# One batch's attention moved into the token mix and output projection of the batch before it

## The chip, the cores and the metric

The kernel runs on one core of a Trainium2 chip. The metric is device time in microseconds (us), median of three runs. The core's engines are TensorE (PE, matrix products), VectorE (DVE), ScalarE (ACT), GpSimd (POOL) and SyncE (SP, which here only issues DMAs). Each engine works through its own list of instructions in order; semaphores tie the lists together.

## The reference

Three stages over 4 batches of 576 tokens, all in fp32:

```
x = softmax(q k^T / 8 + mask) v          # 8 heads of 64; heads 0-3: the last 32 keys,
                                         # heads 4-7: keys of the same class mod 32, causal
h = gelu(x @ w_in); u, v = halves(h)     # 512 -> 512 + 512
v = layernorm(v) * g
x = x + (u * (w_sg @ v + b_sg)) @ w_out  # w_sg mixes the 576 tokens
x = x + relu(layernorm(x) * g2 @ w1) @ w2   # 512 -> 2048 -> 512
```

## The kernel before

Phase A loops over the batches; phase B (the last line above) then runs over six tiles of 384 tokens, for all batches together, and isn't changed. A product is done as three in fp32r (`split_product`, L839 to L841): high by high, high by low, low by high, so that each operand exists as a rounded part (`..._hi`, made by a copy) and a remainder (`..._lo`, made by a subtraction, mostly on POOL).

Phase A for one batch, as PE's list has it:

- Attention, in 22 blocks: a local block has 96 queries and 128 keys, a strided one up to 7 residue classes (126 queries, 126 keys; the last of each pair 72). A block holds the two heads of a pair. `scores` (L857, L858) first adds the mask into PSUM by a bf16 product with the identity, then multiplies the queries, with all 128 rows (two heads of 64), by keys stored twice with zeros in the other head's rows, 256 columns in fp32. `maxima` (DVE, L653) takes both row maxima, `exps` (ACT, L474) the exponentials with row sums, `normalise` (DVE, L660, L664) divides, `transposes` (PE, L869) turns both heads, `copy_pT` (ACT, L485) brings them to SBUF, `values` (PE, L883) multiplies by all 128 columns of v and `copy_low`, `copy_high` (L670, L491) keep the half of each head that is wanted. Queries are scaled by ACT beforehand (L466). Scores run three blocks ahead, and values two blocks behind.
- `v_part`: the v half of w_in, 5 groups of 12 products of 512 columns; then 8 `u` groups, 8 `mix` groups (14 products of 288 columns) and 8 `out` groups (12 of 288). ACT and DVE empty them (`gelu_v`, `gelu_u`, `gate`, `add_out`); DVE and POOL normalise v in between.
- The eight PSUM banks are shared in time: four for scores, two for transposes, two for values; then all eight for the groups.

PE's list for a batch is: attention (the first v products between its last blocks), v, u, mix, out, with the first three score blocks of the next batch between the last out groups. In the last batch, the mean of tile 0 of phase B (`mean_product`, L947) follows the u groups. POOL has summed the four chunks for it by then: it does so (`sum_x`, L368, L372) as soon as the last values product is done, ahead of the v normalisation. SP loads the next batch's q, k and v when a batch's last values product is done.

Of the kernel before, what the change touches and what calls it, by code (L numbers as in the profile page):

```python
# [16 lines left out]
F32 = mybir.dt.float32  # L17
# [6 lines left out]
P = 128  # L24
B, H, S, D = 4, 8, 576, 64
DM = H * D
# [16 lines left out]
CLASSES = P // CLASS  # L43
SB = CLASSES * CLASS
# [8 lines left out]
for _pair in range(PAIRS // 2, PAIRS):  # L53
    for _r in range(0, STRIDE, CLASSES):
        _n = min(CLASSES, STRIDE - _r) * CLASS
        BLOCKS.append((_pair, _n, _n, _r * CLASS, STRIDE + _r * CLASS, 2))
NT = len(BLOCKS)


# [10 lines left out]
GROUP_BANK = [(NT - 4 + i) % 4 for i in range(4)] + [4] + 3 * list(range(8))  # L70
NGELU = NS + 2 * GC
NMIX = 2 * GC
W_PARTS = (slice(0, KC * P), slice(KC * P, KC * P + DM))
NOUT = 2 * KC
WIN_SPLIT = (9, 11, 13, 15)
EARLY = 3
DVE_W2 = (0, 1, 2, 8, 9)


def sequence_block_kernel(nc, qT, kT, vW, w_in, g1, w_sgT, b_sg, w_out, g2, w_ff, masks, eye, out):  # L80
    with ExitStack() as ctx:
# [15 lines left out]
        k_sb = sb("k_sb", [P, PAIRS, 2, KPAD], F32, phase_a)  # L97
        v_sb = sb("v_sb", [P, NT, P], F32, phase_a)
        win_hi = sb("win_hi", [P, KC, 2 * GATE], F32R, phase_a)
        win_lo = sb("win_lo", [P, KC, 2 * GATE], F32R, phase_a)  # L100
        eye_b = sb("eye_b", [P, P], BF16, phase_a)
        mask_b = sb("mask_b", [P, 3, 2 * P], BF16, phase_a)
# [5 lines left out]
        op_hi = sb("op_hi", [P, KC, S], F32R, phase_a)  # L108
        op_lo = sb("op_lo", [P, KC, S], F32R, phase_a)
        stat = sb("stat", [P, 3, 2 * NT], F32, phase_a)  # L110
        neg_max, row_sum, row_inv = (stat[:, i, :].rearrange("p (t h) -> p t h", h=2) for i in range(3))
# [6 lines left out]
        with ExitStack() as raw:  # L118
            win_raw = sb("win_raw", [P, KC, 2 * GATE], F32, raw)

        res_by_chunk = res[:].rearrange("p (c t) -> p c t", c=KC)
        wout_raw = res_by_chunk[:, :, S:S + DM]
        wsg_raw = res_by_chunk[:, :, 2 * S:3 * S]
        wsg_raw_last = res[:, 3 * S:4 * S]
        mask_raw = res[:, BS + 3 * S:BS + 3 * S + 3 * P]
        u_sb = sb("u_sb", [P, GC, S], F32, phase_a)
        vn_hi = sb("vn_hi", [P, NS, GATE], F32R, phase_a)
        vn_lo = sb("vn_lo", [P, NS, GATE], F32R, phase_a)
        gt = sb("gt", [P, 3, HALF], F32, phase_a)

        with ExitStack() as attention:
            probs = sb("probs", [P, 4, 2 * P], F32, attention)
            probsT = sb("probsT", [P, 2, 2 * P], F32, attention)
        gv = sb("gv", [P, 3, GATE], F32, phase_a)
        phase_a.close()

# [31 lines left out]
        s_bank, t_bank, o_bank = bank[0:4], bank[4:6], bank[6:8]  # L168
# [5 lines left out]
        q_scaled = sem("q_scaled")  # L174
        k_zero = sem("k_zero")
# [13 lines left out]
        x_low, x_high = sem("x_low"), sem("x_high")  # L189
        x_hi, x_lo = sem("x_hi"), sem("x_lo")  # L190
        xe_lo = sem("xe_lo")
# [32 lines left out]
        def res_at(b, chunk, first, n, p0=0, p1=P):  # L224

            return res[p0:p1, bass.ds(b * S + (chunk * BS + first), n)]
# [9 lines left out]
        def head_out(b, t, low):  # L236

            pair, nq, _, q0, _, m = BLOCKS[t]
            p0, p1 = (0, D) if low else (D, P)
            src = o_bank[t % 2][p0:p1, 0:nq] if low else o_bank[t % 2][p0:p1, nq:2 * nq]  # L240
            if m != 2:
                return res_at(b, pair, q0, nq, p0, p1), src

            r0, nr = q0 // CLASS, nq // CLASS
            dst = res_at(b, pair, 0, S, p0, p1).rearrange("p (a r) -> p r a", r=STRIDE)[:, r0:r0 + nr, :]
            return dst, src.rearrange("p (r a) -> p r a", a=CLASS)

# [8 lines left out]
        def res_count(b, i):  # L258

            return b * NOUT + (NOUT + 2 + i)  # L260

        def blocks_upto(pair):
            return sum(1 for blk in BLOCKS if blk[0] <= pair)

        @block.sync
        def _(sp):
            def load_qkv(b, first=False):
                for pair in range(PAIRS):
                    sp.dma_start(q_sb[:, pair, :], qT[b, :, pair, :]).then_inc(q_in[pair], 16)
                    if first and pair == 0:  # L270
                        sp.dma_start(mask_raw, masks).then_inc(mask_in, 16)
                        sp.dma_start(eye_f[:], eye).then_inc(mask_in, 16)
                    for h in range(2):
                        rows = slice(D * h, D * h + D)
                        sp.dma_start(k_sb[rows, pair, h, :], kT[b, rows, pair, :]).then_inc(k_in[pair], 16)  # L275
                    blocks = slice(blocks_upto(pair - 1), blocks_upto(pair))
                    sp.dma_start(v_sb[:, blocks, :], vW[b, :, blocks, :]).then_inc(v_in[pair], 16)
# [10 lines left out]
            with sp.Fori(1, B) as b:  # L288
                sp.wait_ge(pv_ready, b * NT)
                load_qkv(b)  # L290


            sp.wait_ge(pv_ready, B * NT)
# [15 lines left out]
        def _(pool):  # L309
# [3 lines left out]
            pool.wait_ge(k_zero, 2)  # L313
            pool.memset(k_sb[0:D, 1:, 1, :], 0.0).then_inc(k_zero, 1)
            pool.wait_ge(k_zero, 3)
            pool.memset(k_sb[D:P, 1:, 0, :], 0.0).then_inc(k_zero, 1)

            def split_weights(part):

                if part < KC:  # L320
                    pool.wait_ge(win_hi_ready, part + 1)
                    lo, raw_, hi = win_lo[:, part, :], win_raw[:, part, :], win_hi[:, part, :]
                else:
                    i = part - KC
                    if i < NS - 2:
                        pool.wait_ge(wrest_hi_ready, i + 1)
                        lo, raw_, hi = wsg_lo[:, i, :], wsg_raw[:, i, :], wsg_hi[:, i, :]
                    else:
                        i -= NS - 2
                        pool.wait_ge(wrest_hi_ready, NS + i + 1)  # L330
                        lo, raw_, hi = wout_lo[:, i, :], wout_raw[:, i, :], wout_hi[:, i, :]
                pool.tensor_tensor(lo, raw_, hi.bitcast(F32), ALU.subtract).then_inc(wa_lo, 1)

            def split_x(b, pair):
                pool.wait_ge(x_hi, b * PAIRS + (pair + 1))
                settle(pool)
                pool.tensor_tensor(op_lo[:, pair, :], res_at(b, pair, 0, S), op_hi[:, pair, :].bitcast(F32),  # L337
# [12 lines left out]
            def split_v(b, s):  # L350
                pool.wait_ge(vnh_ready, b * NS + (s + 1))
                pool.tensor_tensor(vn_lo[:, s, :], gv[:, s % 3, :], vn_hi[:, s, :].bitcast(F32),
                                   ALU.subtract).then_inc(vnl_ready, 1)

            def split_gated(b, i):
                _, c, h = GROUPS[NGELU + i]
                pool.wait_ge(gh_ready, b * NMIX + (i + 1))
                pool.tensor_tensor(op_lo[:, c, h * HALF:(h + 1) * HALF], gt[:, i % 3, :],
                                   op_hi[:, c, h * HALF:(h + 1) * HALF].bitcast(F32),
# [35 lines left out]
            def batch(b, first=False, last=False):  # L395
                if first:
                    for part in range(KC):
                        split_weights(part)
                for pair in range(PAIRS - 1):
                    split_x(b, pair)  # L400
                if last:
                    pool.wait_ge(pv_ready, B * NT)
                    pool.memset(xc[:, 0:P], 1.0 / DM).then_inc(b_const, 1)
# [712 lines left out]
```

## Time and profile before

| | us |
|---|---|
| three runs | 764.59, 765.59, 766.84 (median 765.59) |
| the profiled execution | 764.36 |
| its span, first to last instruction | 761.8 |
| PE busy in the span | 739.5 (97%), mean granted clock 0.996 |
| DVE, ACT, POOL busy | 337.4, 275.0, 198.0 |
| first attention product | 6.56 |
| u products of batch 0 start | 59.3 |
| phase B starts | 352.2 |

Busy time of PE counts the pipelined length of each product, so neighbours overlap: what a product costs is the distance between two starts. The stages can be told by the tiles that a product reads: `k_sb`, `probs`, `probsT` are attention, `win` with 512 columns v, with 288 columns u, `wsg` mix, `wout` out. A half-speed stretch shows in PEclk, and in durations.

### The profile page before, as it was taken

The page shows a single profiled execution, that of the slowest core. Times are in us where ns is not written, and L with a number is a line of the kernel's source. Part 1 is how long each engine was busy: PE and PEld are TensorE (multiplying, and loading weights), DVE is VectorE, ACT ScalarE, POOL GpSimd, SP SyncE. Part 2 cuts the span into 40 slices and gives each one's busy share as a digit, 9 for nine tenths or more (in the row PEclk, how much of TensorE's full clock was granted, in tenths as well). Part 3 has the DMA queues.
Part 4 walks back from the last instruction along what each step waited for, and adds up shares of the span by engine and source line. Part 5 has one row for each costly group of instructions (what it writes and reads, how often), then busy time and mean ns, then how long its engine had stood idle before and what let it go on. Part 6 is the DMA issues. An engine that isn't in the chain of part 4 may idle for free.

```text
span 761.8 us, 12255 instructions
## 1 busy us (share of the span) xinstructions
PE 739.5 (97%) x4400; PEld 693.0 (91%) x4400; DVE 337.4 (44%) x736; ACT 275.0 (36%) x826; POOL 198.0 (26%) x190
## 2 busy tenths in 40 slices
PE   6798999999999999999999999999999999999998
PEld 4578986899679977999999999999999999999998
DVE  5955667635854486675453223223122322222112
ACT  6663458425952386352442122121112211211110
POOL 1518602530124203655434021111302031110000
PEclk9899999999999999999999999999999999999999
DMA  8525000600042001011330100100010010001001
GB/s 254 223 65 141 1 0 1 203 0 0 0 134 69 0 1 51 7 64 68 119 122 18 42 1 1 41 1 1 1 42 1 1 43 1 0 1 42 1 1 41
DMA packets 15227, 34.34 MB, mean 45 GB/s; under 512 B 1872, under 2 KB 5200, under 8 KB 15184
## 3 DMA queue, kind: packets, MB, share of 16 engines
q1 hardware_dynamic: 15184, 33.76, 14.0%
q8 instruction: 27, 0.44, 0.2%
q14 instruction: 16, 0.13, 0.1%
HBM read 29.04 MB, written 4.72 MB: 44 GB/s over the span
## 4 chain that ended last, share of the span: by engine, by line
PE 88%; DVE 3%; issue 3%; ACT 2%; DMA 2%; SPq 1%; POOL 0%; DVEq 0%; ACTq 0%
PE bank L839 26%; PE bank L841 26%; PE bank L840 26%; PE bank L883 3%; PE bank L858 2%; PE bank L869 2%; DMA win_raw<-w_in_dram 1%; ACT probs L474 1%; DVE probs L664 1%; DVE stat L653 1%; PE bank L857 1%; SPq L275 1%; PE bank L942 1%; PE bank L941 1%; DMA w_raw<-w_ff_dram 0%
## 5 line engine op out<-in xcount | busy, mean ns | idle before, releaser
L802 DVE SCALAR_TENSOR_TENSOR hid_lo<-bank,hid_hi 128x384 fp32r<-128x384 f32 x96 | 53.5, 557 | 282.8 <-ACT hid_hi L604 282.8
L604 ACT ACTIVATE hid_hi<-bank 128x384 fp32r<-128x384 f32 x96 | 47.1, 491 | 298.1 <-PE bank L841 298.1
L839 PE MATMUL bank<-xn_hi,w_hi 128*128 128x384 f32 x384 | 129.1, 336 | 1.2 <-DVE res L711 1.2
L840 PE MATMUL bank<-xn_lo,w_hi 128*128 128x384 f32 x384 | 129.5, 337 | 0.0
L841 PE MATMUL bank<-hid_hi,w_lo 128*128 128x384 f32 x384 | 129.5, 337 | 0.0
L839 PE MATMUL bank<-hid_hi,w_hi 128*128 128x384 f32 x384 | 129.4, 337 | 0.0
L841 PE MATMUL bank<-xn_hi,w_lo 128*128 128x384 f32 x384 | 129.2, 336 | 0.0
L840 PE MATMUL bank<-hid_lo,w_hi 128*128 128x384 f32 x384 | 128.9, 336 | 0.0
L474 ACT ACTIVATE probs<-bank,stat 96x128 f32<-96x128 f32 (+2 forms) x176 | 61.7, 355 | 38.3 <-DVE stat L653 36.9
L839 PEld LDWEIGHTS bank<-xn_hi,w_hi 128*128 128x128 f32 x384 | 72.1, 188 | 1.4 <-DVE res L711 1.4
L839 PEld LDWEIGHTS bank<-hid_hi,w_hi 128*128 128x128 f32 x384 | 72.2, 188 | 0.0
L841 PEld LDWEIGHTS bank<-xn_hi,w_lo 128*128 128x128 f32 x384 | 72.1, 188 | 0.0
L840 PEld LDWEIGHTS bank<-hid_lo,w_hi 128*128 128x128 f32 x384 | 72.1, 188 | 0.0
L840 PEld LDWEIGHTS bank<-xn_lo,w_hi 128*128 128x128 f32 x384 | 72.1, 188 | 0.0
L841 PEld LDWEIGHTS bank<-hid_hi,w_lo 128*128 128x128 f32 x384 | 72.0, 188 | 0.0
L858 PE MATMUL bank<-k_sb,q_sb 128*96 128x256 f32 (+2 forms) x176 | 54.2, 391 | 0.0
L664 DVE TENSOR_TENSOR probs<-probs,stat 96x256 f32<-96x256 f32 (+2 forms) x88 | 49.8, 566 | 3.0
L883 PE MATMUL bank<-probsT,v_sb 128*128 128x192 f32 (+2 forms) x176 | 50.2, 371 | 0.6 <-DVE res L670 0.2
L869 PEld LDWEIGHTS bank<-eye_f,probs 96*128 96x128 f32 (+2 forms) x176 | 20.5, 142 | 32.4 <-DVE probs L664 14.4
L392 POOL TENSOR_TENSOR xn_lo<-xc,xn_hi 128x1536 fp32r<-128x1536 f32 x6 | 21.0, 3506 | 103.4 <-ACT xn_hi L544 103.4
L337 POOL TENSOR_TENSOR op_lo<-res,op_hi 128x576 fp32r<-128x576 f32 x12 | 17.1, 1424 | 115.1 <-DVE op_hi L677 115.1
L869 PE MATMUL bank<-eye_f,probs 96*128 96x96 f32 (+2 forms) x176 | 33.6, 273 | 8.4 <-DVE probs L664 4.1
(101 smaller groups left out, 1454.1 us busy)
## 6 DMA issues: line engine op xcount, KB each, us to landing
w_raw<-w_ff_dram SPq DMA_DIRECT2D x16, 512.0 KB, 3.5
k_sb<-kT_dram SPq DMA_DIRECT2D x32, 152.0 KB, 5.0
q_sb<-qT_dram SPq DMA_DIRECT2D x16, 288.0 KB, 5.6
out_dram<-res SPq DMA_DIRECT2D x5, 768.0 KB, 3.9
v_sb<-vW_dram SPq DMA_DIRECT2D x8, 384.0 KB, 4.6
v_sb<-vW_dram SPq DMA_DIRECT2D x8, 320.0 KB, 6.6
win_raw<-w_in_dram SPq DMA_DIRECT2D x4, 512.0 KB, 10.2
res<-w_sgT_dram SPq DMA_DIRECT2D x1, 1152.0 KB, 13.3
```

The source lines that it names most:

```text
L337: pool.tensor_tensor(op_lo[:, pair, :], res_at(b, pair, 0, S), op_hi[:, pair, :].bitcast(F32), ALU.subtract).then_inc(x_lo, 1)
L392: pool.tensor_tensor(xn_lo[h][:], xc[:], xn_hi[h][:].bitcast(F32), ALU.subtract).then_inc(xnl_ready, 1)
L474: last = act.activation(probs[0:nq, t % 4, h * nk:(h + 1) * nk], s_bank[t % 4][0:nq, h * nk:(h + 1) * nk], ACT.Exp, bias=neg_max[0:nq, t, ...
L604: act.activation(hid_hi[:, f % 2, :], h_bank[f % 2][:, 0:TILE], ACT.Relu).then_inc(hh_ready, 1)
L664: dve.tensor_tensor(e, e, inv, ALU.mult).then_inc(probs_ready, 1)
L802: dve.scalar_tensor_tensor(out=hid_lo[:, f % 2, :], in0=h_bank[f % 2][:, 0:TILE], scalar=0.0, in1=hid_hi[:, f % 2, :].bitcast(F32), op0=AL ...
L839: pe.matmul(dst, wh, xh, start=(start and i == 0), stop=False)
L840: pe.matmul(dst, wh, xl, start=False, stop=False)
L841: last = pe.matmul(dst, wl, xh, start=False, stop=(stop and i == n - 1))
L858: pe.matmul(dst, q_sb[:, pair, q0:q0 + nq], k_sb[:, pair, :, k0:k0 + nk], start=False, stop=True).then_inc(scores_ready, 1)
L869: last = pe.transpose(t_bank[t % 2][0:nk, h * nq:(h + 1) * nq], probs[0:nq, t % 4, h * nk:(h + 1) * nk], eye_f[0:nq, 0:nq])
L883: pe.matmul(o_bank[t % 2][:, 0:2 * nq], v_sb[0:nk, t, :], probsT[0:nk, t % 2, 0:2 * nq], start=True, stop=True).then_inc(pv_ready, 1)
```

## The change

Blocks come in twins: 24 blocks (strided ones now hold 6 or 5 classes, 108 or 90 queries), 12 twins of two blocks, three twins to each pair. The attention of batch 0 runs alone ("solo"). The attention of batch b+1 runs within the mix and out groups of batch b, in 14 steps: a step has the scores of twin s, the transposes of twin s-2, a mix or out group, the values of twin s-2, and in two steps a second group. The last batch has its products alone.

Scores are now one product per head and block, with 64 of the array's rows (rows 0 to 63 for one head, 64 to 127 for the other) and 128, 108 or 90 key columns. Values are one product per head and block, with 64 of the array's columns, so each head's result lands in its own half of the partitions. The mask product, the doubled keys, their zeroing, and the scaling of the queries go. Instead DVE does, per head and block, one `tensor_tensor_reduce` from PSUM that adds the mask, scales, writes to SBUF and takes the maximum; and ACT's exponentials read SBUF. The normalisation is four `tensor_scalar` per twin. In the interleaved steps, attention uses banks 0 to 3 (one set) and the groups banks 4 to 7; solo has two sets.

```diff
-            def scores(b, t):
...
-                pe.matmul(dst, eye_b[0:nq, 0:nq], mask, start=True, stop=False)
-                pe.matmul(dst, q_sb[:, pair, q0:q0 + nq], k_sb[:, pair, :, k0:k0 + nk],
-                          start=False, stop=True).then_inc(scores_ready, 1)
+            def scores(b, s, solo=False):
+                if solo and s >= 2:
+                    pe.wait_ge(max_ready, b * NT + 2 * (s - 1))
+                if not solo and s >= 1:
+                    pe.wait_ge(max_ready, b * NT + 2 * s)
...
+                for j in range(2):
+                    pair, nq, nk, q0, k0, _ = BLOCKS[2 * s + j]
+                    for h in range(2):
+                        rows = slice(h * D, (h + 1) * D)
+                        last = pe.matmul(scores_at(s, j, h, solo), q_sb[rows, pair, q0:q0 + nq],
+                                         k_sb[rows, pair, k0:k0 + nk], start=True, stop=True)
+                last.then_inc(scores_ready, 1)
...
+            def values(b, s, solo=False):
...
+                for j in range(2):
+                    for h in range(2):
+                        rows = slice(h * D, (h + 1) * D)
+                        last = pe.matmul(values_at(s, solo)[rows, j * nq:(j + 1) * nq], v_sb[0:nk, 2 * s + j, rows],
+                                         probsT[0:nk, (2 * j + h) * nq:(2 * j + h + 1) * nq], start=True, stop=True)
+                last.then_inc(pv_ready, 1)
```

DVE:

```diff
+            def maxima(b, s, solo=False):
...
+                for j in range(2):
+                    mask = mask_b[0:nq, BLOCKS[2 * s + j][5], 0:nk]
+                    for h in range(2):
+                        last = dve.tensor_tensor_reduce(out=probs_at(s, j, h), in0=scores_at(s, j, h, solo),
+                                                        in1=mask, scale=-SCALE, scalar=3.0e38, op0=ALU.add,
+                                                        op1=ALU.min, accum_out=stat_at(neg_max, s, j, h))
...
+            def normalise(b, s):
...
+                for j in range(2):
+                    for h in range(2):
+                        e = probs_at(s, j, h)
+                        last = dve.tensor_scalar(e, e, stat_at(row_inv, s, j, h), None, ALU.mult)
+                last.then_inc(probs_ready, 1)
```

PE while the next batch's attention is interleaved:

```diff
+            def period(b, first=False):
+                projections(b, first)
+                for s in range(STEPS):
+                    if s < TWINS:
+                        scores(b + 1, s)
+                    if s >= LAG:
+                        transposes(b + 1, s - LAG)
+                    for i in AFTER_T[s]:
+                        group(b, NGELU + i, first)
+                    if s >= LAG:
+                        values(b + 1, s - LAG)
+                    for i in AFTER_P[s]:
+                        group(b, NGELU + i, first)
```

PE in solo, then DVE in solo:

```diff
+            for s in range(STEPS):
+                if LAG <= s:
+                    transposes(0, s - LAG, solo=True)
+                if s < TWINS:
+                    scores(0, s, solo=True)
+                if LAG <= s:
+                    values(0, s - LAG, solo=True)
...
+            for s in range(STEPS):
+                if s < TWINS:
+                    maxima(0, s, solo=True)
+                if 1 <= s <= TWINS:
+                    normalise(0, s - 1)
```

POOL in the last batch:

```diff
+            def last_period(b):
+                split_all_v(b)
+                pool.wait_ge(group_ready, b * len(GROUPS) + NGELU)
+                pool.memset(xc[:, 0:P], 1.0 / DM).then_inc(b_const, 1)
+                pool.memset(eps_c[:], EPS).then_inc(b_const, 1)
+                pool.wait_ge(b_const, 2)
+                pool.tensor_copy(mean_w[:], xc[:, 0:P]).then_inc(b_const, 1)
+                sum_x(0)
+                split_sum(0, False)
```

The v products run batch by batch in one piece, over the four chunks of their input; `gv` and `gt` get a buffer for every group instead of three.

## Rows read from the trace of the kernel before

**Rows 1.** The page's busy time, share of the span and instructions, by engine.

```profile
PE 739.5 (97%) x4400; PEld 693.0 (91%) x4400; DVE 337.4 (44%) x736; ACT 275.0 (36%) x826; POOL 198.0 (26%) x190
```

**Rows 2.** Windows: length, then busy us (instructions) by engine, granted clock, DMA.

```profile
6.56:12.20 5.64, 5.64 (x17) 3.88 (x18) 3.16 (x10) 3.34 (x16) 0.00 (x0) 1.00 1.00 275
...
21.50:25.70 4.20, 2.32 (x13) 1.31 (x11) 4.17 (x9) 2.92 (x13) 1.84 (x2) 1.00 1.04 405
25.70:31.70 6.00, 5.24 (x18) 3.94 (x19) 5.90 (x12) 3.81 (x18) 4.02 (x2) 0.53 0.71 249
...
34.00:42.90 8.90, 6.32 (x34) 4.00 (x33) 8.73 (x24) 6.25 (x28) 5.32 (x3) 1.00 0.00 0
42.90:59.30 16.40, 16.40 (x78) 12.94 (x78) 7.99 (x23) 8.31 (x24) 3.84 (x6) 1.00 0.39 110
59.30:71.90 12.60, 12.60 (x96) 12.58 (x95) 9.62 (x15) 7.18 (x15) 11.26 (x13) 1.00 0.66 168
71.90:74.60 2.70, 0.29 (x3) 0.06 (x1) 0.00 (x0) 0.41 (x1) 2.52 (x2) 1.00 0.00 0
...
186.40:210.50 24.10, 22.94 (x131) 16.05 (x129) 21.57 (x74) 21.61 (x102) 2.80 (x2) 1.00 0.00 0
...
226.90:309.40 82.50, 81.75 (x520) 70.61 (x519) 50.43 (x139) 44.39 (x160) 26.00 (x33) 1.00 0.12 36
```

**Rows 3.** Timeline of PE, batch 1: one local block; columns start us, us, engine, line.

```profile
108.10 0.27 PE L857 MATMUL bank<-mask_b,eye_b 96*96 96x256 bf16 x1
108.21 0.59 PE L858 MATMUL bank<-k_sb,q_sb 128*96 128x256 f32 x2
108.65 0.33 PE L869 MATMUL bank<-eye_f,probs 96*128 96x96 f32 x2
108.81 0.52 PE L883 MATMUL bank<-probsT,v_sb 128*128 128x192 f32 x2
```

**Rows 4.** Timeline of PE, batch 3: the first products of two mix groups.

```profile
322.42 0.29 PE L839 MATMUL bank<-wsg_hi,vn_hi 128*128 128x288 f32 x1
...
324.29 0.29 PE L839 MATMUL bank<-wsg_hi,vn_hi 128*128 128x288 f32 x1
```

**Rows 5.** Timeline of PE, batch 0: from 128 to 64 weight columns in v.

```profile
56.33 0.39 PE L841 MATMUL bank<-win_hi,op_lo 128*128 128x512 f32 x1
56.56 0.40 PE L839 MATMUL bank<-win_hi,op_hi 128*64 128x512 f32 x1
```

**Rows 6.** Timeline of DVE: normalising a block, a scaling, six out groups added.

```profile
105.02 0.15 DVE L660 RECIPROCAL stat<-stat 96x2 f32<-96x2 f32 x1
105.21 0.42 DVE L664 TENSOR_TENSOR probs<-probs,stat 96x256 f32<-96x256 f32 x1
105.55 0.41 DVE L653 TENSOR_REDUCE stat<-bank 96x2 f32<-96x256 f32 x1
...
142.56 0.55 DVE L688 TENSOR_SCALAR gv<-gv,mean_var,rstd_v 128x512 f32<-128x512 f32 x1 [0.16 <-POOL rstd_v L347]
...
346.98 2.27 DVE L711 TENSOR_TENSOR res<-bank,res 128x288 f32<-128x288 f32 x6
```

**Rows 7.** Timeline of ACT: an accumulator read and the operation after it.

```profile
105.40 0.19 ACT L474 ACTIVATION_READ_ACCUMULATOR probs<-bank,stat 96x1 f32 x1
105.49 0.35 ACT L474 ACTIVATE probs<-bank,stat 96x128 f32<-96x128 f32 x1
```

**Rows 8.** Timeline of PE and DVE at the start.

```profile
5.22 1.01 DVE L641 CAST mask_b<-res 128x384 bf16<-128x384 f32 x2 [2.89 <-DMA eye_f<-eye_dram]
6.77 1.06 PE L858 MATMUL bank<-k_sb,q_sb 128*96 128x256 f32 x2
```

**Rows 9.** Timeline of POOL, batch 3: preparing the mean of tile 0.

```profile
301.12 0.20 POOL L403 MEMSET xc<- 128x128 f32 x1 [3.73 <-PE bank L883]
...
304.65 1.01 POOL L372 TENSOR_TENSOR acc<-acc,res 128x384 f32<-128x384 f32 x1 [0.18 <-POOL acc L372]
...
319.28 1.01 POOL L387 TENSOR_TENSOR acc_lo<-acc,acc_hi 128x384 fp32r<-128x384 f32 x1
```

More of the change, by code:

```diff
@@ L272, in load_qkv @@
                         sp.dma_start(eye_f[:], eye).then_inc(mask_in, 16)
[L273 to L276, printed above, removed]
+                    blocks = slice(2 * PER_PAIR * pair, 2 * PER_PAIR * (pair + 1))
                     sp.dma_start(v_sb[:, blocks, :], vW[b, :, blocks, :]).then_inc(v_in[pair], 16)
@@ L393, in split_xn, with split_all_v @@
                                    ALU.subtract).then_inc(xnl_ready, 1)
[L395 to L403, printed above, removed]
-                    pool.memset(eps_c[:], EPS).then_inc(b_const, 1)
-                    pool.wait_ge(b_const, 2)
-                    pool.tensor_copy(mean_w[:], xc[:, 0:P]).then_inc(b_const, 1)
-                    sum_x(0)
+            def split_all_v(b):
                 root_v(b, 0)
@@ L549, in weights_hi, with gelus @@
                     act.activation(w_hi[f][:, part], w_raw[:, f % 2, part], ACT.Copy).then_inc(wff_hi, 1)
[L551 to L561 removed]
+            def gelus(b, first=False, last=False):
                 for s in range(NS):
@@ L598, in _ @@
+            period(0, first=True)
             with act.Fori(1, B - 1) as b:
-                batch(b)
-            batch(B - 1, last=True)
+                period(b)
+            last_period(B - 1)
             def hidden_hi(n, f):
@@ L796, in _ @@
+            round_x(0, PAIRS - 1)
+            period(0, first=True)
             with dve.Fori(1, B - 1) as b:
-                batch(b)
-            batch(B - 1, last=True)
+                period(b)
+            last_period(B - 1)
             def hidden_lo(n, f):
@@ new lines, in transposes @@
+            def transposes(b, s, solo=False):
+                _, nq, nk, _, _, _ = BLOCKS[2 * s]
+                if solo and s >= 2:
+                    pe.wait_ge(pT_copied, b * TWINS + (s - 1))
+                if not solo and s >= 1:
+                    pe.wait_ge(pT_copied, b * TWINS + s)
+                pe.wait_ge(probs_ready, b * TWINS + (s + 1))
+                settle(pe)
+                for j in range(2):
+                    for h in range(2):
+                        cols = slice((2 * j + h) * nq, (2 * j + h + 1) * nq)
+                        last = pe.transpose(transposed_at(s, solo)[0:nk, cols], probs_at(s, j, h), eye_f[0:nq, 0:nq])
+                last.then_inc(pT_ready, 1)
```

600 lines of the change are left out of this document (294 added, 306 removed).

## The prediction

> **What bounds the kernel now.** I read the page's busy line first: PE 97%, DVE 44% [rows 1]. The other engines could be slower without harm as long as PE has work, so the question is what PE does and where it stands still. Windows by stage answer it [rows 2]: a batch in the middle, from u products to u products (226.9 to 309.4), takes 82.5 us, 81.75 of them busy. Its attention stretch (186.4 to 210.5, 24.1 us) is also busy, with ACT and DVE at 21.6 us beside it. So little idle time is there to be filled: of the 82.5 us under 1.5. What the change can save is PE's own work in attention.
>
> That work is what is left when the dense products are taken off. v: 60 products at 0.23 [rows 5] = 13.8; u: 12.6 for its 96 [rows 2]; mix: 8 groups at 1.87 [rows 4] = 15.0; out: 96 like u = 12.6. Together 54.0, so attention costs 82.5 - 54.0 = 28.5 us a batch, stalls included.
>
> **Attention inside a period (three times).** From starts in one block [rows 3]: the mask product 0.11; 256 fp32 columns 0.44, which is 1.7 ns a column; two transposes 0.16. The mask products go. A local twin (two blocks) has 4 score products of 128 columns, 4 x 128 x 1.7 ns = 0.87; 4 value products of 96, 0.65; 4 transposes, 0.32: in all 1.84. A strided twin has 96 columns in the mean: 0.65 + 0.65 + 0.32 = 1.62. Six of each: 20.8 us if the halves of the array take turns. Columns set a product's time, not rows, and there are as many as before; so halving the rows pays only if two halves work at once. If they always do, scores and values halve: 6 x 1.08 + 6 x 0.97 = 12.3 us. No row shows two products at once. I take the middle, 16.5, because a head's products come in its own order (each fp32 product is two instructions), so that only neighbours of different heads can meet.
>
> Between shapes of the array (64 rows, full, 64 columns, and back) there are 4 changes a step, 48 a period. The nearest row has none: going from 128 to 64 weight columns in v, the next product starts after the usual 0.23 [rows 5]. The other end is that the array empties each time: a product of 288 columns lasts 0.29 and the next group's rhythm is 1.87/14 = 0.13 [rows 4], a tail of 0.16. I take 0.05, nearer to the row: 2.4 us; and 1.6 us for waits that come late. So 20.5 us instead of 28.5: 8.0 less a period, 24.0 in three. Bounds: 12.3 (16 less) to 20.8 + 48 x 0.16 + 1.6 = 30.1 (1.6 more).
>
> The Trainium skill, page "TensorE: Matmul & The Clock Gate", section "Part 3: Packing small matmuls — row/col tiling", says products in different row groups run concurrently, and gives 3.07 times for four row tiles. By that the attention would be near 14 us; the trace of before can't show it.
>
> Does PE get its inputs? The steps hold 27.6 us of mix and out, so 27.6 + 20.5 = 48 us of PE in 14 steps, some 3.5 each. DVE in them: the new mask-and-maximum operation, 48 times. Not in the trace; an addition from PSUM of 288 columns takes 2.27/6 = 0.38 [rows 6], so 128 columns about 0.20, plus an accumulator read, for which ACT's is 0.09 from start to start [rows 7]: 0.29, strided 0.26, in all 13.2. Bounds 0.15 (no separate read, two columns at once) and 0.6 (two passes). Normalising: reciprocal 0.19 to the next start, and four scalings; one of 512 columns lasts 0.55 [rows 6], so 128 columns 0.17 to 0.36; I take 0.23 from start to start: 1.1 a twin, 13.2. Copies of results 1.8, rounding 1.7, gates 8 x 0.9 (two operations of 288 columns) = 7.2, out additions 8 x 0.4 = 3.2. Sum 40.3, under 48. ACT has less: per twin four exponentials at 0.35 [rows 7], two copies, near 2. Each wait in a step (transposes for last step's normalising, values for this step's copy behind a group, scores for last step's maxima) is answered a product group earlier. So PE sets the pace here, and DVE could lag a little without harm. v and u in four banks instead of eight lose nothing: ACT is busy 7.2 of the 12.6 us in which the u groups run [rows 2].
>
> **Solo attention (batch 0).** Before, it and v end at 59.3 [rows 2]. In the new order PE issues the transposes of twin s-2 ahead of the scores of twin s, the transposes wait for the normalising that DVE does last in step s-1, and DVE's next maxima wait for those scores. So nothing overlaps in the ring DVE to PE to DVE: maxima 1.1 + normalising 1.1 + PE's 0.32 transposes, 0.65 scores, 0.16 tail, 0.2 for changes and signals = 3.55 us a step. Before, two of the 22 blocks took (42.9 - 6.6)/11 = 3.3 in the mean [rows 2], with scores three blocks ahead. At half clock PE's part doubles by 1.07: 4.6. PE's real share would be (0.32 + 0.65 + 0.5)/3.55 = 41%. The window 21.5 to 25.7, with busy 2.32 of 4.2, was followed by a granted clock of 0.53; one with 6.32 of 8.9 kept 1.00 [rows 2]. So the clock should be low for part of it. Its first products run slow anyway: 1.06 for a pair that later lasts 0.59 [rows 3, 8]. I take 4.1, ten rings = 41.
>
> Start 5.4 (the identity lands at 5.2 [rows 8]; the zeroing and the query scaling that went took no path time but about 1 us), first scores, maxima, exponentials and normalising to 10.5, + 41 = 51.5, + 5.0 for the last two twins' transposes, copies and values, none of which v products fill any more = 56.5, + v 13.8 + 1.5 at half clock = 71.8. Against 59.3: 12.5 more. Bounds: rings of 3.2 (3.5 more) and of 4.9 (21 more). POOL's four remainders of w_in no longer hit DVE's path: they run while DVE waits for PE.
>
> **First mix of batch 0.** PE stands 2.4 of 2.7 us now [rows 2], for POOL's remainders of v and w_sg. With five v buffers the gelus don't wait and the scores come in between: 1.5 less. Bounds 0 to 2.4.
>
> **Last batch.** POOL's sum for tile 0 now waits for all u groups. From memset to sum it was 301.12 to 305.66 [rows 9] = 4.5; ACT's rounding 0.5, signals 0.2, remainder 1.0 [rows 9] = 6.2. PE has `mean_product` next in its list, so everything behind it, mix and out, waits: 6 us that weren't there. After such a stop the clock should be low for a while; the start lost 5.64/2 = 2.8 that way [rows 2]. I take 8.5 in all; bounds 4 and 10. The next stop, var_product before mix 6, has its input after some 10 us, as late as PE gets there.
>
> **Sum.** -24.0 + 12.5 - 1.5 + 8.5 = -4.5 on the profiled execution's 764.4: 759.9. The median of the runs is 1.2 above it: 761. Phase B isn't touched, and its weights land earlier.
>
> **Rivals.**
> 1. Halves overlap fully: attention 12.3 + 2 = 14.3 us, 14 less a period, and rings of 3.2: -42.6 + 3.5 - 1.5 + 8.5 = -32: 733. For it: the two heads' operands share no rows or banks. Against: the order within a head.
> 2. Slower: solo's ring. It stays at half clock with rings of 4.9 and ends 21 later, and periods save 7.0 each: -21 + 21 - 1.5 + 9 = +7.5: 773. For it: the half clock of 25.7 to 31.7, after 55% busy [rows 2]. Against: at half clock PE is at 60% and may rise. It decides once ten rings and the end cost more than the periods save less 7, that is from rings of 4.6 on with 8 a period.
> 3. The halves take turns and each change empties the array (0.16): periods lose 1.6 each, solo another 3: +4.8 + 15.5 - 1.5 + 8.5 = +27: 793. Against it: no loss in [rows 5], though that row may not be such a change. The Trainium skill, page "TensorEngine Tiling (Array Packing)", section "Key Properties", says that changing the tiling mode drains TensorE; that speaks against this change, and no row here shows its price.
> 4. DVE becomes the bound. At 0.6 a mask-and-maximum costs 28.8 a period, DVE's sum 56 against 48: 8 x 3 - 24 = 0 there, solo another 12.5: 25 - 1.5 + 8.5 = +32: 798. It decides from (48 - 27.1)/48 = 0.44 on. Against: the sum above.
>
> **Chances.** Forecast 0.38 (its own range 751 to 770); rival 1 0.19; rival 2 0.20; rival 3 0.12; rival 4 0.11. About 0.3% (2.3 us) is what can be told from no change. Faster: most of the first (0.28), rival 1, a little of rival 2: 0.49. Same: 0.10. Slower: 0.41. The range leaves out the far ends of rivals 1, 3 and 4: 739 to 787.
>
> **What would show it.** Start of u in batch 0 near 72, with PE idle in every solo step waiting for DVE's scaling, and PEclk below 10 there. From u to u in the middle near 74.5 us. Starts of a twin's eight score instructions: 0.87 (turns) or 0.43 (both) in all, and a longer gap at the changes if the array empties. PE standing 6 us ahead of L947's successor in the last batch. Wrong: PE waiting for DVE's maxima inside the periods, a solo under 45 us, or a period above 80.

## The result, and the profile after

The changed kernel takes 767.05 us (median of 20 runs, 765.28 to 769.75), the kernel before 765.62 in the same rounds (20 runs, 764.27 to 766.84): ratio 1.0023, 95% interval 1.0013 to 1.0032. It is slower by 0.1 to 0.3%; the forecast was 761, faster. The profiled executions took 767.55 and 764.36, with spans of 765.8 and 761.8. The table goes by them. They are 3.2 us apart, the medians 1.4; the rest is the scatter of single executions.

| stretch, us | before | after | difference | predicted |
|---|---|---|---|---|
| start to u of batch 0 | 59.3 | 79.5 | +20.2 | +12.5 |
| u of batch 0 to u of batch 3 | 250.1 | 223.8 | -26.3 | -25.5 |
| u of batch 3 to phase B | 42.8 | 52.8 | +10.0 | +8.5 |
| phase B | 409.6 | 409.7 | +0.1 | 0 |
| span | 761.8 | 765.8 | +4.0 | -4.5 |

The busy line of the page after, which answers [rows 1]:

```profile
PE 720.7 (94%) x4744; PEld 681.1 (89%) x4744; DVE 328.5 (43%) x1024; ACT 253.0 (33%) x738; POOL 198.0 (26%) x192
```

PE is busy 19 us less in a span that is 4 longer: it stands still more. Windows of the changed kernel, in the columns of [rows 2], say where:

```profile
11.38:54.50 43.12, 28.82 (x212) 20.97 (x212) 24.67 (x144) 22.97 (x98) 8.05 (x4) 1.00 0.36 137
54.50:60.04 5.54, 0.00 (x1) 0.03 (x1) 5.44 (x4) 0.48 (x1) 5.38 (x4) 1.00 0.00 0
...
155.70:229.60 73.90, 73.72 (x607) 64.95 (x606) 49.40 (x212) 38.33 (x138) 23.33 (x28) 1.00 0.16 56
...
316.00:322.00 6.00, 0.21 (x3) 0.05 (x1) 0.00 (x0) 0.93 (x2) 4.46 (x7) 0.93 0.00 0
322.00:326.00 4.00, 4.00 (x16) 4.00 (x17) 1.75 (x1) 0.94 (x2) 0.14 (x1) 0.50 0.00 0
```

In a middle batch PE is busy 73.72 of 73.90 us, as the plan of the change has it. (The 1.00 in the first row doesn't show it, but products last nearly twice as long there: eight score instructions 1.10 us, in a period 0.61.) The cost is in solo attention, where 54.50 to 60.04 has no product at all while DVE and POOL are both busy, and in the last batch (316 to 322).

**The stop at the end of solo.** Timelines of PE, DVE and POOL of the changed kernel there:

```profile
60.04 0.80 PE L924 MATMUL bank<-eye_f,probs 90*90 90x90 f32 x4 [5.54 <-issue]
63.20 0.77 PE L891 MATMUL bank<-win_hi,xop_hi 128*128 128x512 f32 x1 [0.82 <-issue]
```

```profile
51.28 0.79 DVE L701 TENSOR_SCALAR probs<-probs,stat 90x90 f32<-90x90 f32 x4
...
53.51 6.43 DVE L701 TENSOR_SCALAR probs<-probs,stat 90x90 f32<-90x90 f32 x4
```

The same four, one by one, from shorter windows of the same view:

```profile
53.51 2.37 DVE L701 TENSOR_SCALAR probs<-probs,stat 90x90 f32<-90x90 f32 x1
55.80 1.43 DVE L701 TENSOR_SCALAR probs<-probs,stat 90x90 f32<-90x90 f32 x1
57.16 1.43 DVE L701 TENSOR_SCALAR probs<-probs,stat 90x90 f32<-90x90 f32 x1
58.51 1.43 DVE L701 TENSOR_SCALAR probs<-probs,stat 90x90 f32<-90x90 f32 x1
```

```profile
53.48 2.34 POOL L346 TENSOR_TENSOR win_lo<-win_raw,win_hi 128x1024 fp32r<-128x1024 f32 x1 [5.83 <-DVE win_hi L676]
55.77 4.11 POOL L362 TENSOR_TENSOR xop_lo<-res,xop_hi 128x576 fp32r<-128x576 f32 x3
```

The same four scalings take 0.79 us once and 6.43 the next time. The second set began as POOL's last remainder of w_in did and ended at 59.94, when POOL's three remainders of x were done (59.88). One by one, each scaling starts 0.03 us after one of POOL's four operations (53.48, 55.77, 57.13, 58.48) and ends 0.06 after it: each waits for a whole operation of POOL's, and POOL's next one starts just ahead of DVE's next. The transposes wait for the last scaling.

**A step inside a period** (PE; the attention of batch 1 within the mix groups of batch 0: a mix group ends, values, scores, transposes, the next group begins), and DVE's maxima in it:

```profile
112.08 0.29 PE L1006 MATMUL bank<-wsg_hi,vn_hi 128*128 128x288 f32 x1
112.21 0.29 PE L1007 MATMUL bank<-wsg_hi,vn_lo 128*128 128x288 f32 x1
112.43 0.55 PE L940 MATMUL bank<-probsT,v_sb 128*64 128x96 f32 x8
112.91 0.68 PE L909 MATMUL bank<-k_sb,q_sb 64*96 64x128 f32 x8
113.52 0.55 PE L924 MATMUL bank<-eye_f,probs 96*128 96x96 f32 x4
113.86 0.38 PE L891 MATMUL bank<-wsg_hi,vn_hi 128*128 128x288 f32 x1
```

```profile
110.48 0.28 DVE L688 CUSTOM_DVE_ANT_0 probs<-bank,mask_b 96x128 f32<-96x128 f32 x1
110.69 0.08 DVE L688 DVE_READ_ACCUMULATOR2_ANT stat<- 96x1 f32 x1
110.69 0.28 DVE L688 CUSTOM_DVE_ANT_0 probs<-bank,mask_b 96x128 f32<-96x128 f32 x1
```

Read the starts: eight score instructions 0.61 us (112.91 to 113.52), eight value instructions 0.48, four transposes 0.34. In turns they would be 0.87 and 0.65, with full overlap 0.43 and 0.33: they lie between. At the first change of shape, from the mix product of 112.21 to the values, the next start comes after 0.22 instead of the 0.13 that is usual between products of 288 columns: 0.09. In the kernel before, where the array stays whole, this place has the usual 0.13 (97.37 to 97.50, an out product and then a mask product).

Behind the transposes the first mix product also holds up the next one (0.21, 113.86 to 114.07, as in the step before, 110.39 to 110.61). But transposes and mix both use the whole array, and the kernel before has such a delay too, where no shape changes. Its PE behind a score product:

```profile
97.86 0.48 PE L839 MATMUL bank<-op_hi,wout_hi 128*128 128x288 f32 x1
98.18 0.30 PE L840 MATMUL bank<-op_lo,wout_hi 128*128 128x288 f32 x1
```

0.32 instead of 0.13. So this delay isn't a price of the halves; what makes it stays open. The DVE operation goes from start to start in 0.21, its read under the next one.

**The last batch.** PE of the changed kernel; the second row is the first mix product, which lasts 0.44 us where that of [rows 4] lasts 0.29:

```profile
321.98 0.66 PE L1012 MATMUL bank<-acc_hi,mean_w 128*128 128x384 f32 x1 [5.79 <-POOL acc_lo L412]
...
322.75 0.44 PE L891 MATMUL bank<-wsg_hi,vn_hi 128*128 128x288 f32 x1
...
348.91 0.40 PE L891 MATMUL bank<-gated_hi,wout_hi 128*128 128x288 f32 x1 [2.03 <-DVE res L748]
```

and DVE ahead of that second stop:

```profile
343.69 2.55 DVE L766 RECIPROCAL rstd<-rstd 128x384 f32<-128x384 f32 x1 [0.21 <-ACT rstd L566]
346.28 2.21 DVE L772 SCALAR_TENSOR_TENSOR xc<-xc,g2c,rstd 128x384 f32<-128x384 f32 x4
348.40 1.54 DVE L748 TENSOR_TENSOR res<-bank,res 128x288 f32<-128x288 f32 x4
```

The first stop was predicted. The second wasn't: out groups now have four banks, and DVE's additions, which free them, are queued behind the normalising of tile 0.

### The profile page after: what moved, and what is told of

Read it like the earlier page. It is cut to its first block, busy times and chain, and to the rows that moved or that the text cites. A ratio compares the mean times of both kernels' runs of the same rounds, so it can differ in the third digit from the quotient of the medians.

```text
span 765.8 us, 12852 instructions
## 1 busy us (share of the span) xinstructions
PE 720.7 (94%) x4744; PEld 681.1 (89%) x4744; DVE 328.5 (43%) x1024; ACT 253.0 (33%) x738; POOL 198.0 (26%) x192
## 4 chain that ended last, share of the span: by engine, by line
PE 91%; issue 4%; DVE 3%; ACT 1%; POOL 1%; DMA 1%; SPq 0%; DVEq 0%; POOLq 0%; ACTq 0%
PE bank L891 27%; PE bank L892 26%; PE bank L893 26%; PE bank L909 4%; PE bank L924 3%; PE bank L940 3%; DVE probs L701 1%; DVE probs L688 1%; DMA eye_f<-eye_dram 1%; PE bank L1006 0%; PE bank L1007 0%; DVE rstd L766 0%; PE bank L1012 0%; PE bank L1013 0%; DVE xc L772 0%
## 5 line engine op out<-in xcount | busy, mean ns | idle before, releaser
L501 ACT ACTIVATE probs<-probs,stat 96x128 f32<-96x128 f32 (+2 forms) x192 | 71.9, 378 | 17.4 <-DVE stat L688 17.3
L688 DVE CUSTOM_DVE_ANT_0 probs<-bank,mask_b 96x128 f32<-96x128 f32 (+2 forms) x192 | 41.0, 266 | 37.6 <-PE bank L909 34.6
L701 DVE TENSOR_SCALAR probs<-probs,stat 96x128 f32<-96x128 f32 (+2 forms) x192 | 50.9, 324 | 1.8
L924 PE MATMUL bank<-eye_f,probs 96*128 96x96 f32 (+2 forms) x192 | 29.7, 286 | 23.1 <-issue 17.7
L924 PEld LDWEIGHTS bank<-eye_f,probs 96*128 96x128 f32 (+2 forms) x192 | 19.7, 151 | 30.6 <-issue 26.8
L384 POOL TENSOR_TENSOR gated_lo<-u_sb,gated_hi 128x288 fp32r<-128x288 f32 x32 | 27.0, 846 | 61.8 <-ACT gated_hi L547 61.8
L891 PE MATMUL bank<-wsg_hi,vn_hi 128*128 128x288 f32 x128 | 41.0, 320 | 1.7 <-issue 1.7
```

Of the source, the lines that this page charges most:

```text
L384: pool.tensor_tensor(gated_lo[:, c, cols], u_sb[:, c, cols], gated_hi[:, c, cols].bitcast(F32), ALU.subtract).then_inc(gl_ready, 1)
L501: last = act.activation(probs_at(s, j, h), probs_at(s, j, h), ACT.Exp, scale=-1.0, bias=stat_at(neg_max, s, j, h), accum_out=stat_at(row_s ...
L688: last = dve.tensor_tensor_reduce(out=probs_at(s, j, h), in0=scores_at(s, j, h, solo), in1=mask, scale=-SCALE, scalar=3.0e38, op0=ALU.add, ...
L701: last = dve.tensor_scalar(e, e, stat_at(row_inv, s, j, h), None, ALU.mult)
L891: pe.matmul(dst, wh, xh, start=(start and i == 0), stop=False)
L924: last = pe.transpose(transposed_at(s, solo)[0:nk, cols], probs_at(s, j, h), eye_f[0:nq, 0:nq])
```

## The experiments

My theory (A): the whole loss against the forecast is POOL holding DVE's scalings at the end of solo, and the rest of the sum stands. Each ratio is to the kernel before on the same chip, with its 95% interval. The changed kernel wasn't run beside the variants, and the kernel before took 765.62, 765.25, 764.53 and 764.88 in the four rounds; so a difference to the 767.05 of the changed kernel is uncertain by about 1 us, apart from the scatter.

**x1: POOL's last two w_in remainders and x remainders in turn.**

```diff
-            for pair in range(PAIRS):
-                split_x(0, pair)
+                split_x(0, c)
```

> Only GpSimd's order in the solo attention changes: each remainder of x is made right behind one of w_in, so that two of the three that stood behind the last w_in are done earlier. Theory A (VectorE's four scalings at 53.5 us, 6.43 long instead of about 0.8, are held by GpSimd's work in the same stretch, 53.48 to 59.88): GpSimd's block is then 2.34 + 1.42 = 3.8 us instead of 6.4, the scalings about 3.8, time 2.5 us less than the changed kernel (764.5). Rival B (the scalings are held by something else, the ring's end or ScalarE's exponentials): no change, 767.

Measured 765.70 us, ratio 1.0005 (0.9994 to 1.0017). Its PE and POOL:

```profile
58.66 0.80 PE L923 MATMUL bank<-eye_f,probs 90*90 90x90 f32 x4 [2.97 <-issue]
```

```profile
53.81 2.04 POOL L362 TENSOR_TENSOR xop_lo<-res,xop_hi 128x576 fp32r<-128x576 f32 x1 [4.98 <-DVE xop_hi L714]
55.81 2.34 POOL L346 TENSOR_TENSOR win_lo<-win_raw,win_hi 128x1024 fp32r<-128x1024 f32 x1
```

POOL's block at the last scalings is 4.4 us instead of 6.4, DVE takes 3.86, PE stops 2.97. The time, 1.4 less than the changed kernel, lies between the two expectations (2.5 less and no change): PE's stop got 2.6 shorter, but the rings before it ended 1.2 later (transposes at 53.36, not 52.17), since POOL's moved work now stood beside earlier scalings (the four of 31.55 last 2.41, before the edit 1.24).

**x2: w_in split earlier, and with it the x remainders.**

```diff
-WIN_SPLIT = (5, 7, 9, 11)
+WIN_SPLIT = (4, 5, 6, 7)
...
-            for pair in range(PAIRS):
+                if c == 1:
+                    split_x(0, 0)
+            for pair in range(1, PAIRS):
```

> The w_in parts are rounded in solo steps 4 to 7 instead of 5, 7, 9, 11, and GpSimd's order follows. Theory A: only one remainder of x (1.4 us) is left beside the last scalings; PE's gap of 5.5 us before the last transposes falls to about 1, time 4.5 to 5 less than the changed kernel (762). The two scalings beside w_in remainders in the middle cost 0.3 to 1 each. Rival B: 767.

Measured 762.78, ratio 0.9965 (0.9951 to 0.9980). PE and DVE of this kernel:

```profile
55.26 0.80 PE L926 MATMUL bank<-eye_f,probs 90*90 90x90 f32 x4 [0.20 <-issue]
...
58.42 0.77 PE L893 MATMUL bank<-win_hi,xop_hi 128*128 128x512 f32 x1 [0.82 <-issue]
```

```profile
53.49 1.67 DVE L703 TENSOR_SCALAR probs<-probs,stat 90x90 f32<-90x90 f32 x4
```

With POOL's block 6.4, 4.4 and 1.4 us long the scalings last 6.43, 3.86 and 1.67, and PE stops 5.54, 2.97 and 0.20. The cause of the stop is shown, and what its removal gives: some 4.3 us of the kernel's time (767.05 less 762.78), and with it the changed kernel is 0.2 to 0.5% faster than the kernel before, not slower. From the last ring to v it takes 5.7 us (52.73 to 58.42) instead of 11.0.

**x3: scores ahead of the transposes in solo.** This tests whether the ring that the prediction drew sets a solo step.

```diff
-                if LAG <= s:
-                    transposes(0, s - LAG, solo=True)
                 if s < TWINS:
                     scores(0, s, solo=True)
+                if LAG <= s:
+                    transposes(0, s - LAG, solo=True)
```

> Solo only: TensorE issues the scores of twin s ahead of the transposes of twin s-2. Theory A (the ring VectorE - transposes - scores - VectorE sets 4.1 us a step, and the idle PE in it keeps the clock at its lower level): scores leave the ring, a step falls to 2.4 to 3.0 us, solo ends 12 to 17 us earlier, though the GpSimd block of 6.4 us at its end stays or grows because the w_in remainders crowd together: time 10 to 14 less than the changed kernel, 753 to 757. Rival B (ScalarE's or VectorE's own work sets the step, 4 us whatever TensorE's order): under 3 us less. Rival C: the order helps but the clock stays at the lower level: steps of 3.3, 8 less, 759.

Measured 759.63, ratio 0.9929 (0.9907 to 0.9952): rival C was right. Steps of local twins fell from 4.2 to some 3.5, not to 2.4 to 3.0. PE of this kernel, one step:

```profile
17.63 1.17 PE L909 MATMUL bank<-k_sb,q_sb 64*96 64x128 f32 x8
18.74 0.90 PE L924 MATMUL bank<-eye_f,probs 96*128 96x96 f32 x4
20.32 0.91 PE L940 MATMUL bank<-probsT,v_sb 128*64 128x96 f32 x8 [0.69 <-issue]
21.16 1.17 PE L909 MATMUL bank<-k_sb,q_sb 64*96 64x128 f32 x8
```

Another wait took the place of the one removed: values now stand right behind the transposes and wait 0.69 us for ACT's copy. And PE's own part, 2.8 of 3.5, is at half speed: scores 1.11 instead of 0.61.

**x4: the sum for tile 0 not behind the last u groups.**

```diff
-                split_all_v(b)
-                pool.wait_ge(group_ready, b * len(GROUPS) + NGELU)
+                pool.wait_ge(pv_ready, B * TWINS)
...
+                split_all_v(b)
...
-                gelus(b)
+                gelus(b, last=True)
...
-                sum_hi(0, False)
```

> Last batch only: GpSimd makes the constants and the sum for tile 0 ahead of normalising v, as in the kernel before, waiting for the last values product only. Theory A (the stop of 5.8 us before the mean's product, and the half clock for some 5.5 us after it, are what the last batch lost): 5.8 + 2.5 = 8 less, 759. Rival B (the stop only hides a later wait, as tile 0's normalisation or VectorE falling behind): 3 less or nothing, 764 to 767.

Measured 761.38, ratio 0.9949 (0.9930 to 0.9968). `mean_product` follows at 316.72 without a stop, and PE isn't slowed behind it. That is 5.7 less than the changed kernel, where 8 were expected: part is given back later, on PE:

```profile
342.06 0.61 PE L890 MATMUL bank<-gated_hi,wout_hi 128*128 128x288 f32 x1 [3.21 <-DVE res L747]
```

The wait for DVE's additions grew from 2.6 in two stops (the longer 2.03) to 3.8 in two, and behind the longer one PE is at half speed again (0.24 from start to start; granted clock 0.50 from 342.06 to 347.00). The last batch takes 47.8 us instead of 52.8.

**x5: both heads' scores on rows 0 to 63.**

```diff
-                        rows = slice(h * D, (h + 1) * D)
+                        rows = slice(0, D)
```

> The scores of both heads of a pair read rows 0 to 63 (the second head's scores are then those of the first: that part of the result is left out). Theory A (products in different halves of the rows overlap, which is why eight score instructions take 0.61 us instead of the 0.87 that their columns make): in the periods they take 0.85 to 0.87, a period from u to u 12 x 0.22 = 2.7 us longer. Rival B (0.61 comes from something else, as a cheaper fp32 pass for 64 rows): 0.61 and no change.

One run: 787.10 us, 20 more than the changed kernel. PE of this kernel:

```profile
111.44 1.11 PE L909 MATMUL bank<-k_sb,q_sb 64*96 64x128 f32 x8
112.48 0.55 PE L924 MATMUL bank<-eye_f,probs 96*128 96x96 f32 x4
```

Eight instructions take 1.04 us instead of 0.61, with the same columns, banks and order. So products on different rows do overlap, and it is worth 4.2 us a period (from v to v, the mean of three periods, 79.6 instead of 75.5), more than the 2.7 expected. With 6.8 in solo these make 19.4 of the 20. 1.04 is also more than the 0.87 of columns alone, which I hadn't expected: on the same rows something beyond the columns is paid as well, perhaps the loading of the weights (PEld is busy 0.90 us for the eight instead of 0.47). How much of the overlap is columns and how much is loading isn't separated.

**x6: scores of the next twin between transposes and values.** It avoids both waits of x3.

```diff
+            scores(0, 0, solo=True)
...
-                if s < TWINS:
-                    scores(0, s, solo=True)
+                if s + 1 < TWINS:
+                    scores(0, s + 1, solo=True)
```

> Solo only: scores of twin s+1 stand between the transposes and the values of twin s-2, so they are out of VectorE's ring and cover ScalarE's copy between transposes and values. Theory A (waits in a ring, not work, set the solo step; after x3 the ring was transposes - copy - values, 3.5 us): steps of 2.7 to 2.9 (TensorE's work at the lower clock), 6 to 8 us less than x3, 752 to 754; if TensorE, now without gaps, gets its full clock, steps near 2.3 set by VectorE, 749. Rival B (VectorE's and ScalarE's work sets 3.3 to 3.5): as x3, 759.

Measured 757.22, ratio 0.9901 (0.9884 to 0.9918); v starts at 52.5, not 63.2. PE of this kernel:

```profile
15.14 1.16 PE L909 MATMUL bank<-k_sb,q_sb 64*96 64x128 f32 x8
16.23 0.55 PE L940 MATMUL bank<-probsT,v_sb 128*64 128x96 f32 x8
16.71 0.55 PE L924 MATMUL bank<-eye_f,probs 96*128 96x96 f32 x4
17.19 0.68 PE L909 MATMUL bank<-k_sb,q_sb 64*96 64x128 f32 x8
...
25.63 0.52 PE L924 MATMUL bank<-eye_f,probs 96*128 96x96 f32 x4 [2.35 <-issue]
```

From transposes to transposes the steps are 2.4, 2.6 and 1.8 (from 14.31) until a stop of 2.35 beside POOL's first w_in remainder. From 16.2 to 26.8 PE is at full speed, after it at half. The windows around that point:

```profile
16.20:26.80 10.60, 6.48 (x82) 4.75 (x80) 9.72 (x55) 8.24 (x37) 2.35 (x1) 0.98 0.99 372
26.80:47.00 20.20, 12.13 (x92) 8.77 (x92) 17.52 (x66) 10.99 (x48) 8.88 (x5) 0.50 0.01 2
```

The time missed the expectation of 752 to 754. What stands in the trace is the other stops (1.42, 1.90, 5.55) and the half speed; how much each of them costs wasn't measured.

**x7: x4, with DVE's first out additions ahead of the normalising.**

```diff
-            invert_root(0)
-            normalise_x(0, range(KC))
...
+                    if i == 2:
+                        invert_root(0)
+                    if i == 4:
+                        normalise_x(0, range(KC))
```

> x4 and, in the last batch, VectorE adds out groups 0 and 1 ahead of the reciprocal and 2 and 3 ahead of tile 0's scaling. Theory A (with four banks instead of eight, the out groups stop behind reciprocal and scaling, 3.4 + 0.8 us in x4, 2.0 in the changed kernel): the stops go, 4 less than x4, 757. Rival B (tile 0's normalisation, now later, becomes late for its first product): the gain is given back there, 761.

Measured 758.48, ratio 0.9916 (0.9901 to 0.9932). The stops at the mean and among the out groups are gone, and phase B begins at 347.0. The last batch takes 43.9 us, before 42.8: all of its loss but 1.1 was these stops and the half speed behind them. But rival B came in part. PE of this kernel:

```profile
346.96 0.41 PE L892 MATMUL bank<-xn_hi,w_hi 128*128 128x384 f32 x1 [2.19 <-issue]
```

Tile 0's normalisation is now what comes last: PE stands 2.19 us ahead of phase B (1.23 in the kernel before, 0.55 in the changed one) and goes on 0.1 behind the end of POOL's remainder `xn_lo` (343.40 to 346.85). Behind that stop PE is at half speed for a while, and phase B takes 411.2 instead of 409.7. So x7 gains 2.9 on x4, where 4 were expected; x8 has the same stop (2.18).

**x8: x2, x6 and x7 together.** Their edits are those above.

> All repairs together: the solo order of x6, the w_in parts of x2, the last batch of x7. If they add up: 767 - 14 (solo ring) - 4.5 (GpSimd's block) - 5.7 - 4 = 739. Each w_in remainder now falls on busier steps of VectorE, which can cost 1.3 each, so 739 to 744; over 750 would mean that the parts hide each other.

Measured 745.25 (744.26 to 746.86), ratio 0.9742 (0.9726 to 0.9758): 19 us faster than the kernel before. Against the changed kernel the three had gained 4.3, 9.8 and 8.6 alone, 22.7 in all; together 21.8. So they add up; the expected 739 to 744 was missed by 1.3, because it counted 14 for the order of solo and x6 gained 9.8. DVE and POOL of this kernel show what is left in solo:

```profile
29.44 0.24 DVE L689 CUSTOM_DVE_ANT_0 probs<-bank,mask_b 90x90 f32<-90x90 f32 x1
...
30.32 2.25 DVE L702 TENSOR_SCALAR probs<-probs,stat 108x108 f32<-108x108 f32 x4
```

```profile
29.59 2.35 POOL L346 TENSOR_TENSOR win_lo<-win_raw,win_hi 128x1024 fp32r<-128x1024 f32 x1 [1.16 <-DVE win_hi L677]
```

The maxima, which read a bank, go on in 0.24 while POOL works, and so does the reciprocal of 108x4 at 30.12 (0.17). The scalings, from SBUF to SBUF, get nowhere until POOL is done (31.94) and end 0.6 later, about what three of the four take.

**x9: values given to the column halves by block instead of by head.**

```diff
-                        last = pe.matmul(values_at(s, solo)[rows, j * nq:(j + 1) * nq], ...
+                        half = slice(j * D, (j + 1) * D)
+                        last = pe.matmul(values_at(s, solo)[half, h * nq:(h + 1) * nq], ...
```

> The four values products of a twin go by block instead of by head to the halves of the array's columns, so two neighbours in the list share a half and only the middle pair differs (each result lands in the wrong place: where the heads' outputs belong is what is changed). Theory A (neighbours in different halves overlap in the columns too): eight value instructions take longer than the 0.49 us of the changed kernel, 0.58 to 0.65, so 12 x 0.12 = 1.4 us more a period. Rival B (columns don't overlap, 0.49 is the load and the length of narrow products): 0.49, no change.

One run: 767.44, and the eight value instructions start in 0.48 us in all, as before the edit. So the order of the halves doesn't matter, as rival B said, but whether column halves overlap isn't shown by it. What makes 0.48 of 0.65 stays open.

**x10: all 16 mix and out groups behind the attention.**

```diff
-AFTER_T = [(0,), (1,), (2,), (3,), (5,), ...
-AFTER_P = [(), (), (), (4,), (), ...
+AFTER_T = [()] * STEPS
+AFTER_P = [()] * (STEPS - 1) + [tuple(range(NMIX + NOUT))]
```

> Attention of the next batch keeps its twins, halves and four banks, but all 16 mix and out groups come after it instead of between its steps. Theory A (the new attention leaves TensorE short of work, and only the groups between its steps cover the waits): steps of 3.3 to 4.2 us at the lower clock, 14 steps 46 to 55 us where they add some 22 now, so a period of 100 to 108 us instead of 73.8, in all 80 to 100 us slower than the changed kernel. Rival B (attention is dense as it was in the kernel before, and where it stands matters little): a period of 75 to 80.

One run: 840.38, 73 more than the changed kernel where 80 to 100 were expected; a period takes 98.6 us from u to u in the middle (179.5 to 278.1). Window of this kernel over the attention of the first period (the last 4 us are mix):

```profile
92.00:140.00 48.00, 34.68 (x248) 26.47 (x249) 27.06 (x162) 26.55 (x115) 9.83 (x8) 0.54 0.05 12
```

The twin blocks without the dense groups between them run much like solo: steps of some 3.4 at half speed. In this order of PE's list the twin blocks and halves alone would be 16 us a period slower than the kernel before (98.6 against 82.5), so without the interleaving there is no gain of 8.7. It doesn't follow that the interleaving makes all of it: within it the different rows alone are worth 4.2 (x5), and a better order of the attention by itself, as x6 has it in solo, wasn't tried here.

## Why the prediction was wrong

**Right: what a period saves.** Predicted 8.0 a period with attention at 20.5; u to u became 73.9 and 73.7, so attention costs 73.9 - 54.0 = 19.9. Added up by starts, its products make 16.6 (16.5 was the middle between turns and full overlap) and the rest 3.3 (4.0 for changes and waits). The middle was a choice between two bounds and not derived, so that it came out this near is partly luck; that products overlap at all, x5 shows, with different rows as the cause. The price of a change was taken as 0.05; the one that can be read, from the whole array to the values' halves, is 0.09. The changes between values, scores and transposes can't be read apart from the products, and most steps have three changes, not four, since the scores follow the values directly. Rival 3 (0.16 each, no overlap) didn't come, since there is overlap. The Trainium skill, page "TensorEngine Tiling (Array Packing)", section "Key Properties", says that a change of tiling mode drains TensorE. The row agrees in sign, but 0.09 is less than the 0.16 that the prediction gave for a whole tail.

**Wrong, and hidden in the sum: the first mix.** It was to gain 1.5 and gained nothing. The period from u of batch 0 takes 76.2 us, 2.3 more than the next (73.9); before it took 85.0, 2.4 more than the next (82.6). PE does stop shorter before the first mix (1.66 instead of 2.42), but it then waits 0.18 for DVE's maxima and 0.86 for DVE's scalings (transposes at 101.11). So the three periods' -26.3 is 8.7 or 8.8 each, against 8.0, and 0 instead of -1.5: two errors of opposite sign.

**Right: DVE isn't the bound.** 0.21 a mask-and-maximum, not 0.29, for the read runs beside the next one. Rival 4 needed 0.44.

**Right: the solo ring.** Ten rings were to take 41 us and took 40.8 (11.38 to 52.17), and x3 shows that the order made them: without that order they shrink. That the number fits so well is luck in part. The 4.1 stood for a clock that is low for part of solo; in fact the products are at half speed all through it (eight score instructions of a local twin 1.10 us, not 0.61), for which the prediction's own sum was 4.6, and the maxima took 0.85 a twin instead of 1.1. Rival 2 came near in the sign and in the half speed, but its rings of 4.9 didn't come.

**Wrong: the cover of POOL's remainders, and with it the end of solo.** The step that failed is "POOL's four remainders of w_in no longer hit DVE's path: they run while DVE waits for PE". I costed the end at 5.0 us; it took 11.0 (52.17 to 63.20). For the first three that held nearly: the scalings beside them took at most 0.4 longer (1.24 at 31.53). The last remainder of w_in comes at step 11, and POOL's three of x right behind it, just when DVE has its last scalings and nothing else is left for PE. x1 and x2 vary POOL's block and the scalings follow; with the block nearly gone the end takes 5.7, near the 5.0 of the prediction. The row that says what POOL does to such a scaling was there to be read in the trace of before, and the prediction doesn't use it: the scaling of one block there, in a normalising like that of [rows 6] where it takes 0.42, lasted 2.14 us while POOL's remainder ran from 20.88 to 23.26. DVE and POOL of the kernel before:

```profile
21.39 2.14 DVE L664 TENSOR_TENSOR probs<-probs,stat 96x256 f32<-96x256 f32 x1
```

```profile
20.88 2.38 POOL L332 TENSOR_TENSOR win_lo<-win_raw,win_hi 128x1024 fp32r<-128x1024 f32 x1 [15.15 <-DVE win_hi L647]
```

The Trainium skill, page "SBUF — State Buffer", section "SBUF: two separate sides", calls the port pair that VectorE and GpSimd share an exclusive lock: of a GpSimd operation and a VectorE operation in a two-port mode or with two SBUF inputs, the one that starts first has the pair for the whole instruction. The rows agree: each of the four scalings waits for one operation of POOL's. Half speed into the v products let v end another 1.0 later, and the first transposes came 0.9 later than estimated; PE's first products waited until 6.58 for the identity, which was estimated to be there at 5.2.

**Too small: the last batch.** It lost 10.0 instead of 8.5. The stop (5.8) and the half speed (22 products at 0.24 instead of 0.134, 2.4 us) were as predicted. "The next stop has its input after some 10 us, as late as PE gets there" left out DVE's queue: with four banks, additions behind a reciprocal of 2.55 and scalings of 2.21 stop PE for 2.0. x7 shows it by moving them.

**The sum.** Solo's end +6.0, its start +0.9, its rings -0.2, v +1.0; periods -0.8; last batch +1.5; phase B +0.1: 8.5, all of the distance between -4.5 and +4.0. A gain of 4.5 was the difference between 25.5 saved and 21 spent, so one end of solo that was 6 too short turned the sign; without POOL's block there (x2) the change is a gain, if a small one. My theory (A) was right in the main and not in full: the end of solo is 6.0 of the 8.5, and the other terms erred too.

## What to carry to other kernels

When work is moved into a stage with nothing beside it, go through every engine's queue at the end of that stage: a wait that dense products covered before is now paid in full. If POOL runs long SBUF operations, look in the trace for DVE operations of a form whose duration jumps beside them, and put POOL's work where DVE reads banks or idles; a block of several POOL operations in a row can hold one DVE operation each. An interleaving that pays in the steady state should be costed apart from its first and last turn, since here these took back more than its 26 us, and three small reorderings gave 22 back.

## What the runs showed of the hardware

- Beside a POOL operation of two SBUF inputs, one of DVE's SBUF-to-SBUF scalings lasts until that operation ends (2.37 and 1.43 us beside operations of 2.34 and 1.40), so four last 0.79 us alone and 6.43 beside four operations in a row. The mask-and-maximum, which reads a bank, isn't touched (0.24), and a reciprocal of 108x4 isn't either (0.17).
- fp32 products of 64 rows and 128 columns: 0.61 us for eight instructions if the two heads use different rows, 1.04 if the same, where columns alone would make 0.87 at the 1.7 ns of the kernel before.
- From a whole-array product to one of 64 weight columns the next start comes 0.09 us later than usual (0.22, not 0.13).
- The granted clock of a window can read 1.00 while products last twice as long: 11.38 to 54.50 of the changed kernel shows 1.00, with eight score instructions in 1.09 instead of 0.61. So, against what stands ahead of the prediction, a half-speed stretch does not always show in PEclk; durations are the surer sign of speed.
- PE stayed at half speed in solo with products for 2.8 of 3.5 us a step (x3). In x6 it was at full speed from 16.2 on, after products without a stop from 11.56; it fell back at 26.8, shortly after it had stood for 2.35 us.
